# Scores put between the first and the second group of transposes, and the order of Vector, Scalar and Tensor instructions around them

## The reference

```python
q, k, v: (4, 8, 576, 64)   M_prev: (4, 8, 64, 64)   z_prev: (4, 8, 64)   beta: (8,)
scores = q @ k.T / sqrt(64), causal;  a = softmax(scores);  local = a @ v
phi(x) = where(x > 0, x, exp(x) - 1) + 1
mem_out = (phi(q) @ M_prev) / (phi(q) . z_prev + 1e-6)
g = sigmoid(beta);  attn = g * mem_out + (1 - g) * local
x = attn laid out as (2304, 512)
h = x @ w_in;  x = piecewise(h) @ w_out        # 512 -> 2048 -> 512; 0 below -1, h above 1, (h+1)^2/4 between
h = x @ w_in;  out = (h * sigmoid(h)) @ w_out  # the same sizes
```

## Time and profile before

| | |
|---|---|
| median of 3 runs | 1037.46 us |
| the profiled execution | 1037.46 us, of which the span of its instructions is 1035.7 |
| TensorE busy (matmul) | 1015.5 us, 98% |
| Vector busy | 489.7 us, 47% |
| Scalar busy | 412.2 us, 40% |
| GpSimd busy | 273.9 us, 26% |
| mean granted TensorE clock | 0.999 |

### The profile page before, as it was taken

The page is one execution under the profiler, slowest core; times in us unless marked ns, Lnnn a source line. Parts: engine busy times, 40 slices in busy tenths (PEclk is TensorE's granted clock), DMA queues, the critical chain, the costliest instruction groups (busy, mean ns, idle before and its releaser), DMA issues.

```text
span 1035.7 us, 16398 instructions
## 1 busy us (share of the span) xinstructions
PE 1015.5 (98%) x6256; PEld 930.8 (90%) x6256; DVE 489.7 (47%) x1063; ACT 412.2 (40%) x935; POOL 273.9 (26%) x276
## 2 busy tenths in 40 slices
PE   5999999999999999999999999999999999999998
PEld 3777777779999999999999999999999999999997
DVE  5888888865544444444444443323223233232222
ACT  4777777753323233232332554223222222232222
POOL 6788888868500000000000465000000000000000
PEclk9999999999999999999999999999999999999999
DMA  5544555413200000000000242000000000000000
GB/s 169 146 143 143 146 141 144 123 44 92 72 1 2 1 0 0 0 0 0 1 1 1 82 133 83 1 1 31 1 30 0 0 30 0 31 1 1 31 1 31
DMA packets 30204, 48.02 MB, mean 46 GB/s; under 512 B 3264, under 2 KB 13504, under 8 KB 30144
## 3 DMA queue, kind: packets, MB, share of 16 engines
q1 hardware_dynamic: 27584, 38.81, 12.5%
q0 software_dynamic: 2560, 8.39, 2.8%
HBM read 42.47 MB, written 4.72 MB: 46 GB/s over the span
## 4 chain that ended last, share of the span: by engine, by line
PE 96%; DVE 1%; DMA 1%; POOL 1%; issue 0%; SPq 0%; ACT 0%; POOLq 0%; DVEq 0%; ACTq 0%
PE ps L904 26%; PE ps L903 26%; PE ps L902 26%; PE ps L869 4%; PE ps L797 4%; PE ps L778 3%; PE ps L857 2%; PE ps L846 2%; PE ps L785 1%; DVE probT L639 1%; PE ps L839 1%; PE ps L822 1%; PE ps L782 1%; DMA qraw<-in_qT 0%; PE ps L832 0%; DMA braw<-in_bN 0%
## 5 line engine op out<-in xcount | busy, mean ns | idle before, releaser
L904 PE MATMUL ps<-xparts,W 128*128 128x384 f32 x768 | 257.8, 336 | 0.0
L902 PE MATMUL ps<-xparts,W 128*128 128x384 f32 x768 | 257.6, 335 | 0.0
L903 PE MATMUL ps<-xparts,W 128*128 128x384 f32 x768 | 257.2, 335 | 0.0
L717 DVE TENSOR_TENSOR glo<-act_t,ghi 128x384 fp32r<-128x384 f32 x192 | 110.8, 577 | 220.7 <-ACT ghi L503 220.7
L503 ACT CAST ghi<-act_t 128x384 fp32r<-128x384 f32 x192 | 98.7, 514 | 229.8 <-PE ps L904 210.8
L300 POOL TENSOR_TENSOR W<-stage,W 128x512 fp32r<-128x512 f32 x64 | 83.0, 1306 | 324.7 <-ACT W L545 321.7
L902 PEld LDWEIGHTS ps<-xparts,W 128*128 128x128 f32 x768 | 144.2, 188 | 4.2
L903 PEld LDWEIGHTS ps<-xparts,W 128*128 128x128 f32 x768 | 144.1, 188 | 4.1
L904 PEld LDWEIGHTS ps<-xparts,W 128*128 128x128 f32 x768 | 144.1, 188 | 0.0
L902 PE MATMUL ps<-ghi,W 128*128 128x384 f32 x384 | 128.3, 334 | 0.0
L904 PE MATMUL ps<-ghi,W 128*128 128x384 f32 x384 | 128.3, 334 | 0.0
(11 more groups left out here) (109 smaller groups left out, 1384.5 us busy)
## 6 DMA issues: line engine op xcount, KB each, us to landing
qraw<-in_qT SPq DMA_DIRECT2D x16, 320.0 KB, 3.5
vn<-in_vN SPq DMA_DIRECT2D x16, 320.0 KB, 3.8
kraw<-in_kT SPq DMA_DIRECT2D x16, 288.0 KB, 2.8
qn<-in_qN SPq DMA_DIRECT2D x16, 288.0 KB, 2.8
zb<-in_zN SPq DMA_DIRECT2D x32, 144.0 KB, 4.1
out_x<-ostage SPq DMA_DIRECT2D x18, 256.0 KB, 2.0
stage<-in_moe_w_in POOLq DMA_DIRECT2D x16, 256.0 KB, 3.7
stage<-in_moe_w_out POOLq DMA_DIRECT2D x16, 256.0 KB, 3.1
```

The source lines that it names most:

```text
L717: nc.vector.tensor_tensor(glo[:, f % SLOTS, :], a, ghi[:, f % SLOTS, :].bitcast(F32), ALU.subtract).then_inc(glo_done, 1)
L902: nc.tensor.matmul(dst, w_lo_, x_hi_, start=first, stop=False)
L903: nc.tensor.matmul(dst, w_hi_, x_lo_, start=False, stop=False)
L904: return nc.tensor.matmul(dst, w_hi_, x_hi_, start=False, stop=last)
```

## The change

TensorE: S0 and S1 of the next pair are moved from behind M21 to behind M1, ahead of M20; PHI comes before REST. Vector: the four `rows` steps and the maxima are mixed with the three copies in another order; two of the maxima now stand behind M21's copy and behind M31's copy, and maxima 4 and 5 now stand behind `low_k`. Scalar: the second part of phi comes before M20's copies, two exponentials before M30's copy, and PHI is copied out before REST. Semaphore waits follow: what waited for PHI as the later of the two waits for REST, and the wait for the weighed values stands at PHI.

```diff
-        T_M0, T_M1, T_M20, T_M21, T_M30, T_M31, T_TAIL, T_REST, T_PHI, T_ROW = range(TURNS)
+        T_M0, T_M1, T_M20, T_M21, T_M30, T_M31, T_TAIL, T_PHI, T_REST, T_ROW = range(TURNS)
...
                 empty_first(p)
                 if more:
                     phi_part_1(p + 1)
+                    phi_part_2(p + 1)
                 empty_main(p, T_M20, 2, 0)
-                if more:
-                    phi_part_2(p + 1)
-                empty_main(p, T_M30, 3, 0)
                 if more:
                     exps(p + 1, 0)
                     exps(p + 1, 1)
+                empty_main(p, T_M30, 3, 0)
+                if more:
                     exps(p + 1, 2)
-                else:
+                    exps(p + 1, 3)
+                if not more:
                     split_x(0, 0, 0)
                     split_x(0, 0, 1)
                 empty_tail(p)
                 if more:
-                    exps(p + 1, 3)
+                    exps(p + 1, 4)
                 else:
                     split_x(0, 0, 2)
                     split_x(0, 0, 3)
+                empty_phi(p)
+                if more:
+                    exps(p + 1, 5)
                 empty_rest(p)
-                if more:
-                    exps(p + 1, 4)
-                empty_phi(p)
-                if more:
-                    exps(p + 1, 5)
                 empty_row(p)
...
                     to_x(p - 1)
+                rows(p, 0)
                 empty_second(p)
-                rows(p, 0)
                 rows(p, 1)
+                if more:
+                    maximum(p + 1, 0)
+                rows(p, 2)
+                if more:
+                    maximum(p + 1, 1)
+                rows(p, 3)
                 empty_main(p, T_M21, 2, 1)
-                rows(p, 2)
-                rows(p, 3)
-                if more:
-                    for c in range(6):
-                        maximum(p + 1, c)
+                if more:
+                    maximum(p + 1, 2)
                 empty_main(p, T_M31, 3, 1)
+                if more:
+                    maximum(p + 1, 3)
                 if more2:
                     low_k(p + 2)
                 if more:
-                    maximum(p + 1, 6)
-                    maximum(p + 1, 7)
+                    maximum(p + 1, 4)
+                    maximum(p + 1, 5)
                 if more2:
                     low_q(p + 2)
                 if more:
+                    maximum(p + 1, 6)
                     norms(p + 1, 0)
+                    maximum(p + 1, 7)
                     norms(p + 1, 1)
+                    norms(p + 1, 2)
                     maximum(p + 1, 8)
-                    norms(p + 1, 2)
                     norms(p + 1, 3)
...
             def turn_rest(p):
                 room(p, T_REST)
-                pe.wait_ge(weighed, 2 * p + 2)
...
             def turn_phi(p):
                 room(p, T_PHI)
+                pe.wait_ge(weighed, 2 * p + 2)
...
                 turn_both(p, T_M0, 0)
                 turn_both(p, T_M1, 1)
+                if more:
+                    score(p + 1, 0)
+                    score(p + 1, 1)
                 turn_corner(p)
                 turn_one(p, T_M21, 2, 1)
-                if more:
-                    score(p + 1, 0)
-                    score(p + 1, 1)
...
+                turn_phi(p)
                 turn_rest(p)
-                turn_phi(p)
                 turn_row(p)
```

More of the change, by code:

```diff
@@ L130, in build @@
         TURNS = 10
-        T_M0, T_M1, T_M20, T_M21, T_M30, T_M31, T_TAIL, T_REST, T_PHI, T_ROW = range(TURNS)
-        BY_ACT = [T_M0, T_M20, T_M30, T_TAIL, T_REST, T_PHI, T_ROW]
+        T_M0, T_M1, T_M20, T_M21, T_M30, T_M31, T_TAIL, T_PHI, T_REST, T_ROW = range(TURNS)
+        BY_ACT = [T_M0, T_M20, T_M30, T_TAIL, T_PHI, T_REST, T_ROW]
         BY_DVE = [T_M1, T_M21, T_M31]
@@ L334, in weigh @@
                 if p:
-                    pool.wait_ge(t_full, TURNS * (p - 1) + T_PHI + 1)
+                    pool.wait_ge(t_full, TURNS * (p - 1) + T_REST + 1)
                 nc.gpsimd.tensor_tensor(phs[:, 0:2 * FULL, :], phir[p % 2][:, 0:2 * FULL, :],
@@ L435, in empty_rest @@
                 act.wait_ge(t_full, TURNS * p + T_REST + 1)
-                act.wait_ge(x_free, p + 1)
                 nc.scalar.copy(turned[:, :, MAIN:S],
@@ L441, in empty_phi @@
                 act.wait_ge(t_full, TURNS * p + T_PHI + 1)
+                act.wait_ge(x_free, p + 1)
                 nc.scalar.copy(turned[:, 0, 0:MAIN], ring(T_PHI)).then_inc(ev_act, 1)
@@ L475, in _ @@
                     split_x(0, 0, 3)
-                empty_rest(p)
-                if more:
-                    exps(p + 1, 4)
                 empty_phi(p)
@@ L481, in _ @@
                     exps(p + 1, 5)
+                empty_rest(p)
                 empty_row(p)
@@ L853, in memory @@
                 pe.wait_ge(x_free, p + 1)
-                pe.wait_ge(ev_act, len(BY_ACT) * p + BY_ACT.index(T_PHI) + 1)
+                pe.wait_ge(ev_act, len(BY_ACT) * p + BY_ACT.index(T_REST) + 1)
                 for c0, c1 in ((0, CUT), (CUT, S)):
@@ L880, in _ @@
                 turn_both(p, T_M1, 1)
-                turn_corner(p)
-                turn_one(p, T_M21, 2, 1)
                 if more:
@@ L885, in _ @@
                     score(p + 1, 1)
+                turn_corner(p)
+                turn_one(p, T_M21, 2, 1)
                 turn_one(p, T_M30, 3, 0)
```

## The result

The changed kernel takes 1049.96 us (median of 4, 1049.15 to 1050.35) against 1037.26 for the kernel before beside it: a ratio of 1.012, 95% interval 1.0108 to 1.0134. It is slower by 12.7 us; 20.7 were forecast, in a range from 1045 to 1067. The profiled spans are 1048.3 and 1035.7 us.

A forecast was written before the change was run, and what follows sets the result against it. TensorE was taken to set the attention stage's pace. Thirteen pairs at +1.53 us (19.9), then 0.9, 0.4 and -0.5, sum to 20.7, so 1037.46 becomes 1058 us; forecast 1052 to 1066, range 1045 to 1067.

The forecast's parts named there:

- TensorE's first half, M30, S2 and S3: Early waits filled, but M30 waits for Scalar's copies of M20: M30 and S2 0.09 us late, S3 0.66.
- S4: On TensorE, S4 waits for maxima 4 and 5 behind `low_k`: 1.31 us late per pair, S3's 0.66 included.
- my lower bound of 1.07: S4's lateness in us if `low_k` takes its shortest, 0.75, and nothing stands.
- ROW: After S4, ROW waits for Scalar's 512-wide copy of PHI: 0.22 us more per pair.
- Pair 14: This pair has no `low_k`, so it pays only 0.66 + 0.22 = 0.9 us.
- pair 15: Without scores, it pays only PHI's copy and the `rows` step before M1: 0.4 us.
- pair 0: At TensorE's lower level, S0 and S1 fill a wait longer than themselves: -0.5 us, between -2 and +3.
- (a): Smaller loss: Vector finishes `low_k` and maximum 5 in time, S4 only 0.66 us late; 1050 us, chance 0.12.
- (b): Larger loss: GpSimd's L318 gets in ahead of `low_k`, S4 2.8 us late; 1077 us, chance 0.07.
- (c): Faster: TensorE's waits at M20 and M21 vanish and nothing replaces them; 1029 us, chance 0.08.
- (d): No change: the 0.55 us won in TensorE's first half and the waits cancel; 1037 us, chance 0.04.
- (e): TensorE falls to its lower level, 1.2 GHz, in every third pair; 1088 us, chance 0.04.

The follow-up runs named there:

- the two combined moves: The changed kernel with `low_k` behind maxima 4 and 5 and maximum 3 ahead of M31's copy: 1037.03 us, ratio 1.0007 to the kernel before.

## Why the prediction was right, step by step

**TensorE's first half, M30, S2 and S3** came within 0.02 us of the forecast. The path (S1, M20, Scalar's two copies, M30, M31, Vector's copy, maximum 3) was the right one, and the two combined moves show that it, with S4, is the whole loss but 0.07 per pair.

**S4** was the mis-sized term: 0.95 late, forecast 1.31, and even below my lower bound of 1.07. The mechanism of `low_k` held (it ends about 0.61 after the GpSimd instruction that it meets), but I let GpSimd run only 0.25 earlier than before. It ran 0.82 earlier (2.33 against 3.15 after M0). Of that 0.60 was there at the second of the `rows` steps (1.52 against 2.12): the first now runs ahead of M1's copy and takes 0.17, where it took 0.56 and ended with GpSimd's conversion L311. The rest came because the third and fourth no longer stand behind M21's copy. So `low_k` met nobody and took 0.75. It comes out below even my bound without any standing, 1.07, because a row on Vector reaches into the next one: the instruction behind maximum 3 began 0.34 after it and the one behind `low_k` 0.67, where I had added the whole 0.42 and 0.75. (The sum for S4 also left out the 0.05 of the semaphore that its bounds have.)

**ROW** was 0.16 later behind S4, forecast 0.22. I did not expect that the stretch from ROW to the next M0 would shrink by 0.13 to 0.15; the kernel with PHI alone shows both belong to this swap, which nets nothing. Together S4 and the tail make 0.97 per pair instead of 1.53.

**The sum.** From the M0 of pair 1 to that of pair 14 the changed kernel goes from 34.95 to 217.46, the kernel before from 35.37 to 205.35: 12.5 us more over thirteen pairs. Pair 14 paid 0.6 (forecast 0.9), pair 15 nothing (forecast 0.4), pair 0 gave 0.4 back (forecast 0.5). That last agreement is luck: in the one profiled execution of each other kernel with scores moved, pair 0 gave back 0.9 to 2.7.

**The rivals.** The measured time is below the 1052 to 1066 that had most of the chance, and inside the range because that was drawn to hold most of rival (a). It is that of (a), 1050, but not by its way: S4 did wait for maximum 5 and was 0.95 late, not 0.66. Of the signs named ahead, the waits at M30, S3 and ROW came as said; the one at S4 was 0.32 (0.6 to 0.9 said), `low_k` 0.75 (1.1), the pair 14.04 (14.6). (b) did not happen, since GpSimd's next instruction began after `low_k` and was the one to stand. (c) and (d) fail on the four new waits. (e) happened only in pair 0, below. The Trainium skill (SBUF — State Buffer, "Who interferes with whom") says that when a Vector instruction with two SBUF inputs and a GpSimd instruction that reads SBUF meet, the one that came first keeps the other out. The traces agree in both directions: L318 took 2.00 where it began 0.02 behind `low_k`, and `low_k` took 1.10 where it came into L318.

## What to carry to other kernels

With a ring of two buffers, work moved ahead of a turn is taken away from between that turn and the one two later; ask what hid the copy before, and move only half if both ends need cover. An in-order engine that feeds the bottleneck has to be read for what each piece of the bottleneck waits on: what is lost at a wait early in the chain need not be waited again at the next one, so removing one of two waits in a row gives little (0.33 or 0.18 us per pair here) and removing both gives more than their sum (0.89). A duration in a profile may be mostly standing, and is then no price to carry to another place.

## What the hardware did that I had not expected

In pair 0 TensorE rose to its upper level (2.4 GHz) sooner and fell again: M20's first three transposes took 0.55 at 18.62, before the change 0.90 at 19.18. (The granted clock of the kernel before reads 1.00 there all the same, so it does not show the lower level in that stretch.) The windows of the changed kernel (stretch, length, busy PE, PEld, DVE, ACT, POOL, clock, DMA):

```profile
18.60:22.40 3.80, 1.67 (x13) 1.17 (x11) 3.70 (x15) 2.93 (x9) 3.69 (x6) 0.93 0.66 167
22.50:28.30 5.80, 5.78 (x24) 4.26 (x25) 4.68 (x13) 2.08 (x7) 5.64 (x5) 0.50 0.60 199
28.50:34.90 6.40, 6.16 (x69) 4.72 (x67) 3.88 (x8) 4.28 (x13) 5.31 (x7) 0.98 0.44 135
```

In a stretch in which TensorE was busy for 1.67 of 3.80 us the clock fell, and it was 0.50 (1.2 GHz) for the almost 6 us of dense work behind. Pair 0 gained only 0.4 us for all that S0 and S1 filled. With the scores alone moved the granted clock from 22.50 to 28.30 was 0.80, and pair 0 gained 2.1. How much of the 1.7 between them is the fall's, no run separates. The clock also differs between executions: the changed kernel's mean granted clock went from 0.993 to 1.000, and at 1.000 it took 1049.6 to 1050.0 us, no less than at 0.997. In the later pairs waits of 0.3 to 0.7 us, four to a pair, did not bring the lower level back.
